# A fused delta-rule attention and two mixture layers: gate data carried in the scattered row, and the scatters tied to the read-out

## The reference, cut to what matters

```python
# 1. recurrent attention, B=4 H=8 S=768 D=48
for t in range(S):
    y[:, :, t] = q[:, :, t] @ state
    state += beta_t * outer(k_t, v_t - state^T k_t)        # k normalised
x = y.transpose(0, 2, 1, 3).reshape(3072, 384)
# 2. one expert of 8 for each token (D=384, F=1024)
logits = x @ w_gate;  e_idx = argmax(logits);  gate_w = softmax(logits)[e_idx]
eom = sigmoid(x @ w_output_gate)
out[mask_e] = gate_w * eom[:, e] * (relu(x[mask_e] @ w1[e]) @ w2[e])
# 3. every token through 4 experts, weighted by its domain shares
p = domain_probs / (domain_probs.sum(-1) + 1e-9)
out = sum_e p[:, e] * (relu(x @ w1[e]) @ w2[e])
```

## Time and profile before

| what | value |
|---|---|
| median of 3 runs | 1532.44 us (1527.02 to 1536.73) |
| the profiled execution, its own time | 1532.27 us |
| its span in the trace | 1530.2 us |
| attention, to the last scatter | about 0 to 374 us |
| layer 2's passes | about 383 to 715 us |
| layer 3 | about 710 to 1530 us |
| mean granted PE clock | 0.961 |

### The profile page before, as it was taken

The page is one execution under the profiler, slowest core; times in us unless marked ns, Lnnn a source line. Parts: engine busy times, 40 slices in busy tenths (PEclk is TensorE's granted clock), DMA queues, the critical chain, the costliest instruction groups (busy, mean ns, idle before and its releaser), DMA issues.

```text
span 1530.2 us, 37591 instructions
## 1 busy us (share of the span) xinstructions
PE 1450.9 (95%) x14905; PEld 1397.5 (91%) x14906; DVE 682.9 (45%) x1422; ACT 349.1 (23%) x856; POOL 252.6 (17%) x138
## 2 busy tenths in 40 slices
PE   5799999997698999999999999999999999999997
PEld 5788888987587999999999999999999999999997
DVE  5476767645654555554443333333333333333332
ACT  2445454432111111012331111111111111111111
POOL 1001010002527233135002002020020010200122
PEclk6899999979798999999999999999999999999999
DMA  6445444332503233304001001000010010000011
GB/s 133 101 96 110 107 104 96 83 110 90 182 21 106 96 103 103 103 21 127 1 0 42 0 0 41 0 23 19 0 41 0 0 41 0 0 0 0 31 46 46
DMA packets 99934, 85.01 MB, mean 56 GB/s; under 512 B 60480, under 2 KB 88384, under 8 KB 99840
## 3 DMA queue, kind: packets, MB, share of 16 engines
q1 hardware_dynamic: 77648, 48.09, 12.8%
q10 hardware_dynamic: 18352, 25.99, 5.3%
q0 software_dynamic: 3840, 9.54, 1.7%
HBM read 67.76 MB, written 15.83 MB: 55 GB/s over the span
## 4 chain that ended last, share of the span: by engine, by line
PE 89%; DVE 3%; DMA 3%; SPq 1%; ACT 1%; issue 1%; another core or an unknown queue 1%; ACTq 0%; POOL 0%; POOLq 0%; DVEq 0%
PE bank L788 23%; PE bank L790 23%; PE bank L789 23%; PE bank L564 12%; PE bank L679 2%; PE bank L822 2%; PE bank L682 2%; PE bank L699 1%; DMA kq_sb<-in_kq_dram 1%; ACT R L925 1%; PE bank L795 1%; PE bank L690 1%; SPq L365 0%; PE bank L856 0%
## 5 line engine op out<-in xcount | busy, mean ns | idle before, releaser
L1112 ACT ACTIVATE gTh<-bank 128x384 fp32r<-128x384 f32 x256 | 126.1, 492 | 640.1 <-PE bank L790 639.1
L1510 DVE SCALAR_TENSOR_TENSOR gTl<-bank,gTh 128x384 fp32r<-128x384 f32 x256 | 142.7, 557 | 269.0 <-ACT gTh L1112 269.0
L788 PE MATMUL bank<-v2h,gTh 128*128 128x384 f32 x768 | 258.5, 337 | 0.0
L790 PE MATMUL bank<-v2h,gTl 128*128 128x384 f32 x768 | 256.8, 334 | 0.0
L789 PE MATMUL bank<-v2l,gTh 128*128 128x384 f32 x768 | 256.6, 334 | 0.0
L790 PE MATMUL bank<-x2T,v1l 128*128 (+1 forms) x768 | 256.5, 334 | 0.0
L788 PE MATMUL bank<-x2T,v1h 128*128 (+1 forms) x768 | 256.5, 334 | 0.0
L789 PE MATMUL bank<-x2T,v1h 128*128 (+1 forms) x768 | 256.5, 334 | 0.0
L1523 DVE SCALAR_TENSOR_TENSOR y_all<-bank,aux_all,y_all 128x384 f32 x168 | 96.3, 614 | 244.7 <-PE bank L790 244.7
L789 PEld LDWEIGHTS bank<-v2l,gTh 128*128 128x128 f32 x768 | 144.2, 188 | 0.0
L788 PEld LDWEIGHTS bank<-v2h,gTh 128*128 128x128 f32 x768 | 144.2, 188 | 0.0
(11 more groups left out here) (192 smaller groups left out, 2135.2 us busy)
## 6 DMA issues: line engine op xcount, KB each, us to landing
w_raw<-in_moe_w_dram ACTq DMA_DIRECT2D x14, 1536.0 KB
v_raw<-in_moe_w_dram SPq DMA_DIRECT2D x14, 768.0 KB, 4.5
xs_in<-x_rows SPq DMA_DIRECT2D x31, 192.0 KB
kq_sb<-in_kq_dram SPq DMA_DIRECT2D x28, 192.0 KB, 2.9
kt_sb<-in_kt_dram SPq DMA_DIRECT2D x24, 196.0 KB, 3.6
vt_sb<-in_vt_dram SPq DMA_DIRECT2D x24, 192.0 KB
kq_sb<-in_kq_dram SPq DMA_DIRECT2D x14, 256.0 KB, 4.3
x_rows<-zeros SPq DMA_DIRECT2D x12, 192.0 KB, 2.9
```

What stands on the lines that cost most here:

```text
L788: pe.matmul(dst, lh, rh, start=first, stop=False)
L790: return pe.matmul(dst, ll, rh, start=False, stop=last)
L1112: act.activation(gTh[:, f, :], bank[f][:, 0:BN], ACT.Relu).then_inc(g_hi, 1)
L1510: dve.scalar_tensor_tensor(out=gTl[:, f, :], in0=bank[f][:, 0:BN], scalar=0.0, in1=gTh[:, f, :].bitcast(f32), op0=ALU.max, op1=ALU.subtract)\
```

## The change

A row of `x_rows` grows from 384 to 406 columns: behind the token's 384 values come its 16 logits, a key that names the chosen expert, its 4 normalised domain shares and its token number. The table `aux_rows` with its 24 scatters, the read-back and `scaled` are gone.

- POOL copies the shares into `rows_st` ahead of each chunk's scatter (`shares_taken`); ACT puts the logits there and DVE the key. `shares_normalized` moves from the last chunk to chunk 0.
- POOL scatters chunk c-2 only when `read_out(c, 0)` is done (`read_mm` at 2c+1). SP's `load_k(c+4, 0)` moves ahead of the wait for the same event.
- The values of chunk 0 are scaled by one POOL instruction and not by 16 of ACT.
- Pass 0 reads no table: its rows are 128 to 256, its expert 0. SP issues one block of zero rows, then pass 0's rows, then its other three blocks. PE waits for `slots_ok` behind `hidden_turned(0)`.
- In each pass DVE adds the row's last 22 columns to `aux_all` (in `turned`), and SP's next row load waits for that (`aux_ok`).
- The gate chain moves behind the last pass: its two exponentials stand on ACT behind `rectified(0)` of layer 3, and DVE's chain behind the low parts of the first block's next tiles (`shares_scaled`). The gate weight is multiplied into the shares.
- POOL's low parts and casts are cut into pieces of 384 or 512 columns.

```diff
@@ widths and POOL in attention
-    x_rows = nc.dram_tensor("x_rows", [NE * REG, DM], f32).ap()
-    aux_rows = nc.dram_tensor("aux_rows", [N, AW], f32).ap()
+    KEY = DM + 2 * NE
+    RW = KEY + E2 + 2
+    x_rows = nc.dram_tensor("x_rows", [NE * REG, RW], f32).ap()
             def rows_out(c):
                 pool.wait_ge(pos_ok, c + 1)
+                pool.wait_ge(shares_ok, c + 1)
...
+            def shares_taken(c):
+                if c >= NST:
+                    pool.wait_ge(scattered[c % NST], 16 * NP * (c // NST))
+                pool.tensor_copy(rows_st[:, c % NST, :, KEY + 1:KEY + 2 + E2], p_sb[:, NP * c:NP * c + NP, :]).then_inc(shares_ok, 1)
...
+            pool.wait_ge(vt_in[0], 32)
+            pool.wait_ge(length_ok, 1)
+            pool.tensor_tensor(vt_sb[:, 0], vt_sb[:, 0], length[:, 0].unsqueeze(2).to_broadcast([128, NPAIR, D]), ALU.mult).then_inc(vt_ok, 2)
+            pool.wait_ge(p_ok, 1)
             for c in range(NC):
-                rows_out(c)
+                shares_taken(c)
+                if c >= 2:
+                    pool.wait_ge(read_mm, 2 * c + 1)
+                    rows_out(c - 2)
+            rows_out(NC - 2)
+            rows_out(NC - 1)
             for e in range(1, NE):
-                low_part(w_raw1[:], w1h[:, e % 2], w1l[:, e % 2], w1_hi, w1_split, e + 1)
-                low_part(w_raw2[:], w2h[:, e % 2], w2l[:, e % 2], w2_hi, w_ready, e + 1)
-                if e in (1, 2):
-                    pool.wait_ge(aux_ok, 1)
-                    for t in range(NT // 2 * (e - 1), NT // 2 * e):
-                        aux_scattered(t)
+                low_part(w_raw1[:], w1h[:, e % 2], w1l[:, e % 2], w1_hi, w1_split, e + 1, 2)
+                low_part(w_raw2[:], w2h[:, e % 2], w2l[:, e % 2], w2_hi, w_ready, e + 1, 1)
@@ SP
+                if c + 4 < NC:
+                    load_k(c + 4, 0)
                 sp.wait_ge(read_mm, 2 * c + 1)
                 expert_ahead(c, 1)
-                if c + 4 < NC:
-                    load_k(c + 4, 0)
...
             sp.wait_ge(tail_ok, 1)
-            for e in range(0, NE, 2):
+            tail_rows(sp, 0)
+            sp.wait_ge(front_zero, 16 * NE)
+            sp.wait_ge(first_zero, 16)
+            for i in range(NST):
+                sp.wait_ge(scattered[i], 16 * NP * (NC // NST))
+            load_rows(x_rows[128:256, :])
+            for e in range(2, NE, 2):
                 tail_rows(sp, e)
             sp.wait_ge(slots_ok, 1)
-            sp.wait_ge(front_zero, 16 * NE)
-            sp.wait_ge(tail_zero, 16 * NE)
-            for i in range(NST):
-                sp.wait_ge(scattered[i], 16 * NP * (NC // NST))
-            load_rows(0)
+            sp.wait_ge(tail_zero, 16 * (NE - 1))
             with sp.Fori(1, NPASS) as s:
                 sp.wait_ge(xsT_mm, s)
-                load_rows(s)
+                sp.wait_ge(aux_ok, s)
+                row = sp.value_load(pass_i[0:1, 3, bass.ds(s, 1)], min_val=0, max_val=NE * REG - 128)
+                load_rows(x_rows[bass.ds(row, 128), :])
@@ ACT
-            values(0, 0)
-            values(0, 1)
...
-            for t in range(BT):
-                scaled(t)
             for t in range(BT):
                 tokens_hi(t)
             for blk in range(NBLK):
                 more = range(BT * (blk + 1), min(BT * (blk + 2), NT))
-                for t in more:
-                    scaled(t)
                 rectified(blk)
+                if blk == 0:
+                    exponents()
@@ DVE
                 dve.tensor_tensor(xsTl[:], src, xsTh[:].bitcast(f32), ALU.subtract).then_inc(xsT_lo, 1)
+                aux = aux_all[:, bass.ds(pass_tile(s), 1), :].rearrange("p o d -> p (o d)")
+                dve.wait_ge(xs_load, 16 * (s + 1))
+                dve.tensor_tensor(aux, aux, xs_in[:, DM:RW], ALU.add).then_inc(aux_ok, 1)
...
             hidden(0)
-            dve.wait_ge(exp_ok, 1)
-            link(dve.tensor_reduce(se, e_l, AX.X, ALU.add))
-            link(dve.tensor_scalar(gw, se, 1e-9, None, ALU.add))
-            link(dve.reciprocal(se, gw))
-            link(dve.tensor_scalar(sig, e_g, 1.0, None, ALU.add))
-            link(dve.reciprocal(e_g, sig))
-            link(dve.tensor_tensor(sig, e_g, hot_f, ALU.mult))
-            link(dve.tensor_reduce(eo, sig, AX.X, ALU.add))
-            dve.tensor_tensor(aux_tok[:, :, 0], se, eo, ALU.mult).then_inc(aux_ok, 1)
...
                 for t in turned:
                     tokens_lo(t)
+                if start and blk == 0:
+                    shares_scaled()
```

More of the change, by code:

```diff
@@ L125, in fused_kernel @@
         minus_gain = place("minus_gain", [128, NC, NPAIR])
-        rows_st = place("rows_st", [128, NST, NP, DM])
+        rows_st = place("rows_st", [128, NST, NP, RW])
         xT_gate = place("xT_gate", [128, KD, NP, 128])
@@ L158, in fused_kernel @@
         w2l = place("w2l", [128, 2, KF, DM], f32r)
-        xs_in = place("xs_in", [128, DM])
+        xs_in = place("xs_in", [128, RW])
         xsTh = place("xsTh", [128, KD, 128], f32r)
@@ L835, in down, with both @@
                 ins.then_inc(y_mm, 1)
-            pe.wait_ge(slots_ok, 1)
+            def both(s):
+                up(s)
+                tokens_turned(s + 1)
+                down(s - 1)
+                hidden_turned(s)
             tokens_turned(0)
@@ L841, in _ @@
             hidden_turned(0)
+            pe.wait_ge(slots_ok, 1)
             with pe.Fori(1, NPASS - 1) as s:
-                up(s)
-                tokens_turned(s + 1)
-                down(s - 1)
-                hidden_turned(s)
+                both(s)
             up(NPASS - 1)
@@ L1274, in shares_normalized @@
             def shares_normalized():
[L1275 removed]
+                shares = p_sb[:, :, 0:E2]
                 dve.wait_ge(p_in, 16)
@@ L1363, in _ @@
                     constants_ranked()
+                    shares_normalized()
                 if c + 4 < NC:
@@ L1487, in _, with both @@
             dve.wait_ge(y_ok, 1)
-            with dve.Fori(1, NPASS - 1) as s:
+            def both(s):
                 relus(s)
@@ L1492, in _ @@
                 hidden(s)
+            with dve.Fori(1, NPASS - 1) as s:
+                both(s)
             relus(NPASS - 1)
```

130 lines of the change are left out of this document (70 added, 60 removed).

## The result

| | before | changed | ratio, 95% interval |
|---|---|---|---|
| median, 13 runs each | 1528.4 us (1525.0 to 1538.4) | 1512.2 us (1505.0 to 1524.9) | 0.9883, 0.9852 to 0.9915 |
| the profiled execution, its span | 1530.2 us | 1503.3 us (its own time 1505.5) | |

The change brings 16 us, not 50: faster by just over 1%, and outside the range of 1470 to 1505. The changed kernel also varies by 20 us, where the kernel before varies by 13; its profiled execution is one of its fastest, so the balance of the two spans shows 27 us of gain.

What follows compares the result with a forecast made beforehand. Layer 3 is PE-bound without gaps, so gains lie ahead of it: attention, between the layers, layer 2's passes. 1.2 + 20.6 + 4.0 + 28.2 - 1.9 = 52.1 off 1532.3 gives 1480, said as 1482; range 1470 to 1505.

Steps and rivals of the forecast that it cites:

- Ahead of chunk 0: Before attention's chunks: PE's key wait ends 2.3 us earlier, shares_normalized costs 1.1; net gain 1.2 us, bounds 0 and 2.3.
- Chunks 1 to 10: Attention: scatters tied to the read-out put PE's stops under gates_product, where they hide; gain 20.6 us.
- The first rival: Attention: the stops move and stay, meeting read_out(c, 1); gain 0 to 10 us, say 1500 us; chance 0.27.
- The chunk from 303.47: Late attention chunk, 28.36 us at clock 0.75 before: 5.0 us gain, between 1.3 (stops alone) and 7.
- Between the layers: Before layer 2: pass 0's rows earlier, first products at full clock, pass 1's rows late; net gain 4.0 us, bounds 1 and 5.5.
- Three long passes: Layer 2: passes of 21.56, 16.43 and 18.73 us become 9.50 without gate chain and 32-byte scatters; gain 28.2 us.
- Each pass: Layer 2: DVE's 22-column addition and the later row load cost nothing; bound 1 us in each of seven passes.
- Layer 3: Layer 3's start: exponentials ahead of ACT's cast make PE wait 1.9 us; loss 1.9, bounds 0 and minus 4.
- The stops' cause: Attention: PE's 0.4 us stops come with POOL's scatters, read as instructions reaching PE late while the scatters' descriptors run.

Runs made afterwards that it cites:

- r2: The changed kernel, unchanged, run again for another profile: 1513.0 us at the upper level; its profiled execution took 1517.3 us.
- r1: The kernel before, unchanged, run again for its profile: 1534.7 us at the upper level, 1.0036 of itself.
- e6: The changed kernel with the scatters of chunks 0 to 9 left out, replaced by a one-column POOL write: 1491.4 us at the upper level.
- e10: The changed kernel with split row load, ACT's first weight load behind pass 1's rows, and scatters tied to ACT's copy: 1481.0 us, 0.9701 of before, upper level.
- e7b: The changed kernel with split row load and ACT's first weight load behind pass 1's rows: 1495.9 us, 0.9783 of before, upper level.
- e3: The changed kernel with the row load split, only the small 22-column load waiting for DVE's addition: 1502.3 us, 0.9843 of before, upper level.
- e5: The changed kernel with POOL's layer 2 low parts uncut, one instruction a matrix: 1527.3 us, 1.0238 of before, lower level.
- e7: The same kernel as e7b (split row load, ACT's later first weight load), in another set: 1482.3 us, 0.9930 of before, lower level.
- e1: The changed kernel without POOL's wait for the read-out ahead of the scatters: 1524.1 us, 0.9948 of before, upper level.

## Why the prediction was wrong

The terms missed by +1.1, -11.7, -7.1, -9.3 and +1.9 us in the profiled execution, which took 1505.5 us. None of them takes the time out of the range of 1470 to 1505 by itself; three losses together do. The median lies 7 us higher still. By r2's profile that is attention, which gains 3 us there and not 9, the passes, and the first 100 us.

*Ahead of chunk 0*: 2.3 us, predicted 1.2. PE's wait for the keys of the earlier trace rows ends at 59.74 and not at 62.48, so the gain of the values is there. The start of the first `gates_product` varies by more: 103.3 in r2 and 104.4 in r1, both with ten microseconds at clock 0.50 before it, against 102.6 and 100.3. So whether `shares_normalized` cost its 1.1 us can't be told.

*Chunks 1 to 10*: 8.9 for 20.6, and this is the step that failed: the place to which the tie moves the stops. That they come with the scatters and cost what I said held: without scatters chunks take 24.0 to 24.9 us (e6), and with the scatter half a microsecond later 24.0 to 25.1 (e10). The place was wrong. I wrote that the stops begin "some 2 us behind POOL's first scatter" and so fall under `gates_product`. The stop that I showed began 2.4 us behind it (148.44 less 0.42, and 145.61), but the timelines of PE in the kernel before have another ahead of it, and that of its weight loads (PEld) a third, shorter one:

```profile
147.67 0.35 PE L564 MATMUL bank<-delta,kt_sb 64*64 64x48 f32 x5 [0.40 <-issue]
```
```profile
146.95 0.20 PEld L564 LDWEIGHTS bank<-delta,kt_sb 64*64 64x64 f32 x4 [0.19 <-issue]
```

They began 1.66 and 1.15 us behind the scatter. `level16_right`, "about 2 us", starts 0.46 us ahead of the tied scatter and so would end 1.5 us behind it, later with a stop in it. The first stops fall into it. I compared two rounded times where a half microsecond decided. The first rival (0.27, "say 1500") named the outcome, "the stops move and stay", but for products behind the six and not ahead of them, and its 1500 left out the two losses below.

*The chunk from 303.47*: 27.7 us at clock 0.84, predicted 5.0 less than 28.36. Without scatters it took 24.0 (e6), nearly the 23.4 predicted, but in e10 26.8. So its loss is the scatters', and at this level no place tried saved it.

*Between the layers*: -3.1 for +4.0. The first half was right in kind: pass 0's transposes came 2.5 us earlier, predicted 3.5, and at full clock. The loss was mis-sized: I had pass 1's rows "half to one and a half us" late, and they were 7.5. I had followed SP's zero blocks but not who else waited for pass 0's rows: ACT, with 3 MB behind that wait. The blocks and the weights then shared the DMA engines, busy for a share of 0.85 over 369.04 to 382.71. e7b gets 6.4 us back by one wait, 9 by the ratios.

*Three long passes*: 28.2 predicted, and all three are gone. That PE's wait named the chain holds; the chain and the 32-byte scatters weren't tried one by one.

*Each pass*: 0 predicted, with a bound of 1 us in each of seven; it cost 7.3 us in the profiled execution, and 6 to 10 in the median (e3). I put the load behind a weight load "just in time", as two delays that add up: issued at 3.0, through at 5.4 or, with one piece of the low part, 6.5. They can be one event: where the piece that holds the addition is the last before the weight load, the rows come second, at 4.7 us and through at 10.8. Where the addition takes 0.5 or 0.8 us, the rows come first and the pass stays at 9.57. The Trainium skill, GPSIMD Engine Reference, Key points, speaks of a contention between POOL and DVE for their shared SBUF interfaces; the trace agrees with 1.50 us for an addition of 0.18, and 2.56 in e5. The estimate of one piece, 1.1 us, was too low: beside pieces of 384 columns, of 0.98 us each, the addition took 2.94 us in r2's profile and 3.95 in e7's, three and four of them, and ended with POOL's last. Besides, a PE that waits pays more than the wait: 1.28 us of "issue", then products at the lower clock. And an undisturbed pass takes 9.57 us, not 9.50, some 2 us over the loop. Its products are spaced slightly wider; why isn't settled.

*Layer 3*: PE's wait was 1.66 us, predicted 1.9. But the stretch to the end didn't grow, as the span ends 7.8 us behind PE's last product, where it ended 9.8 us behind in the kernel before (r1 and r2 show the same 9.8 and 7.8). The trace shows no instruction in that difference; what it is stays open.

*The stops' cause.* They come with the scatters (e1, e6), at the upper level and hardly at the lower one. I had read them as instructions that reach PE late. The page of the changed kernel lists a DMA queue that brings instructions, the larger of two; that it is PE's is inferred:

```profile
q8 instruction: 76, 1.25, 0.4%
```

That is 16 KB a packet. The Trainium skill, Runtime: NRT & Kernel Launch, Instruction fetch mechanics, says that an engine's instructions are refilled in 16 KiB blocks through its own DMA queue; the trace agrees in size. That PE stops because such a block waits behind a scatter would be the simple reading, but the trace of the kernel before speaks against it. In chunk 5 PE stops from 201.49 to 201.91 and from 202.26 to 202.68. These are all the queues that moved a packet from 200.4 to 203.8:

```profile
q1 hardware_dynamic: 1457, 0.21, 46.5%
q0 software_dynamic: 128, 0.39, 33.1%
```

The 128 packets of q0 are a scatter's. No block of instructions came, and yet PE stopped and went on twice, so neither stop ended with the landing of a block. What ends them, and why they hardly come at the lower level, stays open.

## What to carry to other kernels

When a stall is to be hidden under a long instruction, take its delay and the place from the same timeline, to a tenth of a microsecond: here 0.5 us of place were worth 15 us, at the upper level. When an event is brought forward, list everyone who waits for it, not only the one it is meant for: here ACT's weight loads went with the rows. And a small load that hangs on a small operation should not stand in the same queue slot as a large one that the same event lets go; splitting it off took 6 to 10 us and half of the spread away.

## What was not expected of the hardware

- The kernel before takes 1491 to 1494 us in some sets of runs and 1527 to 1529 in others, and the changed one 1489 and 1512 to 1513; in the changed one's profiles most of the difference is in attention, where PE's stops of 0.4 us are there or not. A gain of 1.2% at one level is none at the other.
- A wait of PE of 1.08 us in the loop was followed by 1.28 us in which it waited for nothing named. In the changed kernel's profile that gap isn't in the passes without a wait; but in e7b and e10 a gap of 1.31 and 1.29 us stands at the same place in the loop's first pass, where PE didn't wait for rows. Its cause is open.
- DVE's addition over 22 columns (0.18 us alone) took up to 3.95 us beside POOL's pieces of 384 columns, of 0.98 us each, and up to 2.60 beside instructions of 6.8 us. Cutting an instruction of POOL's doesn't mean that DVE gets in at the first cut.
